# Attention and two MLPs on one core: from whole batches beside the first MLP to one half batch beside each half of it

## What is computed

```python
scores = q @ k.T / 8 + slope[h] * -|i - j|          # only 0 <= i - j < 128, the rest is masked
attn   = exp(scores - max) / (sum + 1e-9)
x      = attn @ v, heads side by side               # (4, 576, 512)
xn     = (x - mean) / sqrt(var + 1e-6) * g_ln
x      = x + relu(xn @ w_ch1) @ w_ch2               # 512 -> 2048 -> 512
h      = relu(x @ w_in)                             # 512 -> 1024
out    = (h * sigmoid(conv3(h))) @ w_out            # conv3: three taps along the positions
```

## Time and profile before

| | |
|---|---|
| median of three runs | 839.34 us |
| the profiled execution, its own time | 845.15 us |
| its span, first to last instruction | 843.4 us |
| mean granted clock of TensorE | 0.990 |
| busy: TensorE, VectorE, ScalarE, GpSimd | 812.5, 521.1, 371.9, 177.3 us |
| instructions | 17148 |
| chain that ended last | TensorE 80%, issue 9%, VectorE 7%, ScalarE 2%, GpSimd 1% |

### The profile page before, as it was taken

One profiled execution on the slowest core, in us unless ns is written; L12 is line 12 of the kernel. 1 busy time (PEld: TensorE's weight loads), 2 busy tenths in 40 slices (PEclk: granted clock), 3 DMA queues, 4 the chain that ended last, 5 costly groups with the idle time before them and its releaser, 6 DMA issues.

```text
span 843.4 us, 17148 instructions
## 1 busy us (share of the span) xinstructions
PE 812.5 (96%) x5871; PEld 770.4 (91%) x5871; DVE 521.1 (62%) x1420; ACT 371.9 (44%) x1031; POOL 177.3 (21%) x170
## 2 busy tenths in 40 slices
PE   9999877999989999998999999999999999999998
PEld 5668776999979999998999999999998999999998
DVE  2556665777447777745677764422228977788862
ACT  4626543566323556522466541222325544444442
POOL 5437772122012112101022110011110110111100
PEclk9999999999989999999999999999999999999999
DMA  5415432222031222112212301411212022221201
GB/s 145 121 45 155 129 85 85 71 74 67 3 120 38 63 72 72 37 58 67 65 50 57 100 9 57 136 57 41 88 52 85 22 79 84 77 77 35 70 23 43
DMA packets 56111, 59.30 MB, mean 70 GB/s; under 512 B 24800, under 2 KB 43232, under 8 KB 55520
## 3 DMA queue, kind: packets, MB, share of 16 engines
q1 hardware_dynamic: 56032, 58.30, 23.4%
HBM read 44.12 MB, written 14.16 MB: 69 GB/s over the span
## 4 chain that ended last, share of the span: by engine, by line
PE 80%; issue 9%; DVE 7%; ACT 2%; POOL 1%; ACTq 0%; DVEq 0%; POOLq 0%
PE bank L1303 22%; PE bank L1305 20%; PE bank L1304 20%; PE bank L1274 3%; PE bank L1242 3%; PE bank L1256 3%; PE bank L1203 2%; PE bank L1194 2%; PE bank L1227 2%; PE bank L1216 1%; PE bank L1286 1%; DVE q_st L1054 1%; PE bank L1295 1%; ACT prob L744 1%; DVE prob L966 1%
## 5 line engine op out<-in xcount | busy, mean ns | idle before, releaser
L1303 PE MATMUL bank<-xn_hi,wa_hi 128*128 128x288 f32 x512 | 158.1, 309 | 3.4 <-issue 1.9
L1303 PE MATMUL bank<-h_hi,wb_hi 128*128 128x288 f32 x512 | 158.3, 309 | 0.5 <-DVE ch_stage L1034 0.5
L1304 PE MATMUL bank<-xn_lo,wa_hi 128*128 128x288 f32 x512 | 152.7, 298 | 0.0
L1305 PE MATMUL bank<-xn_hi,wa_lo 128*128 128x288 f32 x512 | 152.4, 298 | 0.0
L1304 PE MATMUL bank<-h_lo,wb_hi 128*128 128x288 f32 x512 | 151.7, 296 | 0.0
L1305 PE MATMUL bank<-h_hi,wb_lo 128*128 128x288 f32 x512 | 151.5, 296 | 0.0
L1023 DVE SCALAR_TENSOR_TENSOR h_lo<-bank,h_hi 128x288 fp32r<-128x288 f32 x128 | 58.3, 455 | 120.2 <-ACT h_hi L774 118.8
L774 ACT ACTIVATE h_hi<-bank 128x288 fp32r<-128x288 f32 x128 | 52.5, 410 | 176.2 <-PE bank L1305 175.3
L1303 PEld LDWEIGHTS bank<-xn_hi,wa_hi 128*128 128x128 f32 x512 | 97.6, 191 | 7.3 <-issue 5.0
L1303 PEld LDWEIGHTS bank<-h_hi,wb_hi 128*128 128x128 f32 x512 | 97.2, 190 | 4.5 <-issue 2.9
L1304 PEld LDWEIGHTS bank<-xn_lo,wa_hi 128*128 128x128 f32 x512 | 97.8, 191 | 0.0
(11 more groups left out here) (127 smaller groups left out, 1721.3 us busy)
## 6 DMA issues: line engine op xcount, KB each, us to landing
w_stage<-w SPq DMA_DIRECT2D x32, 256.0 KB, 2.9
k_raw<-qkT SPq DMA_DIRECT2D x48, 144.0 KB, 2.9
q_raw<-qkT SPq DMA_DIRECT2D x48, 144.0 KB, 2.9
x_in<-x_spill SPq DMA_DIRECT2D x8, 580.0 KB, 4.4
ch_in<-ch_spill SPq DMA_DIRECT2D x8, 580.0 KB, 5.3
x_spill<-xT SPq DMA_DIRECT2D x4, 1152.0 KB, 4.2
ch_spill<-ch_stage SPq DMA_DIRECT2D x32, 144.0 KB, 2.1
out<-out_stage SPq DMA_DIRECT2D x32, 144.0 KB, 1.8
```

What stands on the lines that cost most here:

```text
L1303: nc.tensor.matmul(dst, w_h, a_h, start=start, stop=False)
L1304: nc.tensor.matmul(dst, w_h, a_l, start=False, stop=False)
L1305: last = nc.tensor.matmul(dst, w_l, a_h, start=False, stop=stop)
```

## The change

Each phase holds one chunk's MLP (16 steps, 32 slots) and one chunk's attention, always the next one:

| phase | MLP | attention |
|---|---|---|
| prologue | none | batch 0, chunk 0 (plain float32, as before) |
| first | batch 0, chunk 0 | batch 0, chunk 1 (now split) |
| loop of 3 passes: one | batch b, chunk 1 | batch b + 1, chunk 0 |
| zero | batch b + 1, chunk 0 | batch b + 1, chunk 1 |
| last | batch 3, chunk 1 | none |

Core of the diff (the functions are rewritten to take batch and chunk):

```diff
-FRAME = {("PT", "A"): 0.0, ("S", "A"): 1.0, ("PT", "B"): 1.01, ("S", "B"): 2.0, ("O", "A"): 3.0, ("S", "C"): 4.0, ("O", "B"): 5.0}
-FIRST_NORM, FIRST_HEAD, HEAD_SLOTS, LAST_NORM = 0.0, 6.5, 5.2, 55.5
-STEPS = 2 * F1
+STEPS = F1
+TILES = ([(128, 0, 128, 128, 0), (128, 0, 256, 0, 128), (64, 128, 192, 0, 384)],
+         [(128, 0, 256, 0, 0), (128, 128, 256, 0, 256)])
+GROUPS = ([[(0, 0), (1, 128)], [(2, 0)]], [[(0, 0), (1, 256)]])
+PARTS = ([(0, 128, 0, 256, 0), (1, 128, 256, 192, 128), (2, 64, 448, 64, 256)],
+         [(1, 128, 128, 256, 0), (0, 128, 0, 128, 0), (2, 128, 384, 128, 128)])
+HEAD0, HEAD_SLOT = 0.9, 2.6
+AT = {("S", 0): 0.0, ("S", 1): 1.1, ("PT", 0): 2.95, ("O", 0): 4.35}
+D_NORM = (1.8, 1.4)
+PREP_AT, PREPV_AT = 1.5, 2.0
+NORM_AT = 24.2
+NORM_TIMES = {("IN", 0): 0.0, ("IN", 1): 1.0, ("OUT", 0): 2.8, ("IN", 2): 3.3, ("OUT", 1): 4.2, ("OUT", 2): 5.2}
-WARM = [(1.79, 8)] + [(m + 0.78, 4) for m in range(2, H)] + ...
+WARM = [(1.79, 8)] + [(m + 0.78, 3) for m in range(2, H)] + ...
-W_PROLOGUE = 8
-FIRST_W, W_SLOTS, W_PACE = 0.9, 1.15, 0.85
+W_PROLOGUE = 10
+FIRST_W, W_SLOT, W_PACE = 0.9, 0.95, 1.1
...
+    if kind != "last":
+        c = ATT_C[kind]
+        out += head_items(c, HEAD0, HEAD_SLOT, AT) + norm_items(NORM_AT, NORM_TIMES)
+        out += [(HEAD0 + HEAD_SLOT * (h - 1) + PREP_AT if h else -0.95, ("PREP", h)) for h in range(H)]
+    if kind == "first":
+        out += [(0.25 + W_PACE * (n - W_PROLOGUE), ("W", n)) for n in range(W_PROLOGUE, NW1)]
...
+        def phases(run, eng):
+            run("prologue", None, 0)
+            run("first", 0, 0)
+            with eng.Fori(0, B - 1) as b:
+                run("one", b, b + 1)
+                run("zero", b + 1, b + 1)
+            run("last", B - 1, None)
...
+            def load_qk(b, c, h):
...
+                sp.dma_start(qk_raw[:, h % 2, :, 0:KEYS[c]], qkT[b, h, :, :, KEY0[c]:KEY0[c] + KEYS[c]]).then_inc(qk_loaded[h % 2], 16)
...
+                sp.dma_start(ch_dram[b, :, :, CH * c:CH * (c + 1)], ch_stage[:]).then_inc(ch_spilled, 16)
...
+            def prob_t_hi(b, c, h):
...
+                nc.scalar.activation(pt_hi[:], bank_of(b, c, ("PT", h, 0))[:], ACT.Copy).then_inc(pt_hi_ready, 1)
...
+                    delays = [("Y", 0.5, "y"), ("PREP", 0, "qk_hi"), ("PREPV", 0, "v_hi"), ("S", 0.4, "exps"), ("PT", 0.3, "pt"),
+                              ("O", 0.3, "o"), ("OUT", 0.3, "norm"), ("A", 0, "relu"), ("B", 0, "evac"), ("W", 0, "w")]
...
+                    delays = [("Y", 0, "y"), ("PREP", 0.1, "q_lo"), ("S", 0.2, "min"), ("S", D_NORM[ca or 0], "normalise"), ("PT", 0.5, "pt"),
+                              ("O", 0.4, "o"), ("IN", 0.2, "stats"), ("IN", 1.1, "apply"), ("OUT", 0.6, "norm_lo"),
+                              ("A", 0.1, "relu"), ("B", 0, "evac"), ("W", 0.3, "w")]
```

1265 lines of the change are left out of this document (528 added, 737 removed).

## The result

The changed kernel takes **892.17 us** (median of 4, 889.37 to 892.98) against 840.13 us for the kernel before on the same chip: a ratio of 1.061, 95% interval 1.058 to 1.065. I had said 849 (815 to 868). The direction was right, the loss was forecast at a fifth of its size (9.7 us of 52), and the time lies outside the range.

The account below looks back on a forecast made before the run. TensorE's own work plus its waits was taken as the bound: floor 806.8 + 19.2 + 7.2 + 12.8 + 3.5 + 3.6 = 853.1 us on the span, put at 849 on the median, slower by 1.2%; range 815 to 868.

Parts of the forecast that it names:

- The prologue: Stage before the first MLP: six fillers off -1.7, early score group off -1.0, two more weight tiles nothing; 56.8 us (56 to 60).
- (a): Chunk-0 phases: the queues' closed chain of waits takes 7.1 us a head against TensorE's 6.3; +19.2 us (0 to 31).
- (f): Transfers on SP: fewer per head and spill, queries loaded two heads ahead; no TensorE wait expected, nothing added to the sum.
- (b): Chunk-1 phases: only outputs now and then wait for pt_lo behind a relu, 0.3 us a head; +7.2 us (0 to 19).
- (c): First phase: GpSimd without slack, VectorE's normalise beside its low parts, 1.6 us a head; +12.8 us (3 to 27).
- (d): Phase ends: next phase's input stands 0.75 slot behind the last head's outputs; 7 x 0.5 = +3.5 us (0 to 10).
- (e): Loop edges: two back edges instead of one, 1.8 us each; +3.6 us against the 1.8 taken out of the floor.
- The third rival: Narrow f32r matmuls are dear: 0.13 us more on four matmuls of 32 chunk-1 heads, +17; 866 us median; chance 11%.
- The queues keep up: Rival: (a) and (b) vanish and the first phase costs 10.4; 820 us median, faster by 2.3%; chance 31%.

Follow-up runs that it names:

- r3_slot28: Changed kernel with heads 2.8 instead of 2.6 slots apart and norms 1.6 slots later; chunk-0 phases 3.5 us longer, chunk-1 phases 6.6 longer, first phase 5.5 shorter.
- r5_s1_early: Changed kernel with a chunk-0 head's second score group right behind the first (0.05 instead of 1.1 slots); three chunk-0 phases 247.2 us instead of 250.6.
- r7_s1_q_pt: Changed kernel with second scores right behind the first, queries' copy before keys' high part, transposes 0.35 and outputs 0.25 slot later; three chunk-0 phases 233.0 us instead of 250.6.
- l1_weights_first: Changed kernel with the second load of the second MLP's input behind five more weight-tile loads; last phase 50.8 us instead of 55.7, ratio interval 1.039 to 1.050.
- c3_combined: r7_s1_q_pt with chunk-0 normalisation at 1.0 slots, eight prologue weight tiles 1.15 heads apart and the edit of l1_weights_first; 850.0 us, ratio interval 1.007 to 1.013.

## Why the prediction was right or wrong

Three terms of the sum failed. The prologue's two more tiles were put at nothing, and six fillers counted as time to be had back: +10.9 us. The ring (a) was right in its mechanism and too short: 0.8 us a head over TensorE's own work, measured 1.44, +18.2 for the three phases. And (f), the transfers, stands in the sum at nothing: +4.6.

**What bounds the kernel** was read rightly: TensorE's own work, plus what it waits for. The three forecast waits (probabilities, low part of the transposes, sum of the outputs) are among those listed; the scores' wait for the low half of the queries I had only inside the ring.

**The prologue: the step failed in its sign.** I took six fillers off at 1.13 us for four and said that "ScalarE and GpSimd have room, so nothing is added" for two more tiles. The fillers are not idle time that can be had back: with three instead of four and tiles closer together the granted clock fell in nine of twelve profiles, and the prologue took 60.8 to 67.9 us: 3 to 11 us lost for the 1.7 saved. With the clock up the prologue is 56.4 to 57.8, against my 56.8. The bounds, 56 to 60, left that state out altogether, though the earlier trace rows had a lower clock in plain sight (0.97 in batch 0's run) and I had named it there.

**(a), the chunk-0 ring: right mechanism, size off.** Ring 7.74 us and not 7.1. The parts that I had summed to 6.85 are there, 0.14 longer in all (normalise 1.49 for my 1.3, the way from the first minima to pt_hi 1.33 for 1.2, the others a little shorter). What was too small is the share of the relus. I added 0.25; in the rows above one low part takes 0.37 in line (344.58 to 344.95) and one high part holds the second exp back by as much (its minima end at 348.26, it starts at 348.63), 0.75 together. Over the floor the ring makes 1.44 a head, 34.6 for 24 heads, where I had 19.2; the phases lost 250.6 - 3 x 70.5 = 39. Even my upper bound, 1.3 a head with "all relus in the ring", was too low. I also took the sum as the pace of the kernel and did not see that TensorE's own places form part of the ring; r3_slot28, r5_s1_early and r7_s1_q_pt showed that.

**(b), chunk-1 phases: right by two errors.** 73.6 us against my 73.05. But the floor under it was wrong. TensorE, a chunk-1 head of the changed kernel, groups that nothing holds up, first instruction of the group and of what follows:

```profile
264.29 0.28 PE L1013 MATMUL bank<-k_hi,q_st 128*128 128x256 f32 x1
...
264.75 0.29 PE L1071 MATMUL bank<-h_hi,wb_hi 128*128 128x288 f32 x1
...
265.55 0.60 PE L1028 MATMUL bank<-ident,prob 128*128 128x128 f32 x4
265.90 0.38 PE L1071 MATMUL bank<-xn_hi,wa_hi 128*128 128x288 f32 x1
...
293.34 0.35 PE L1047 MATMUL bank<-pt_hi,v_st 128*128 128x256 f32 x1
...
293.66 0.22 PE L1047 MATMUL bank<-pt_hi,v_st 128*128 128x128 f32 x1
...
294.05 0.35 PE L1071 MATMUL bank<-h_hi,wb_hi 128*128 128x288 f32 x1
```

0.46 + 0.35 + 0.71 = 1.52 a head. I had 1.95, from durations in the chain of waits (0.73, 0.55, 0.67), which for scores and transposes include the tail that the next group covers. So the floor of such a phase is 51.05 + 8 x 1.52 + 2.1 (six norm groups of 0.35) = 65.3 and not 69, and it lost 8.3 us and not the 4 that I forecast. The chunk-0 head was right by the same accident: 0.63 + 0.68 + 0.86 = 2.17 in the trace, where I had subtracted that 1.95 from a 4.1 that had waits of its own in it: from start to start the groups of a whole head take 3.47 us in the loop of before (scores 0.47, 0.47 and 0.18, transposes 0.35 and 0.68, outputs 0.66 twice). Over the 32 chunk-1 heads that is 14 us of floor too much, and 14 us of waiting too little. With this floor the changed kernel had more to give than I thought, and lost more.

**(c), the first phase**: +2.5 on 82.3, near by the same two errors: over its floor of 65.3 the phase lost 19.5 us, where I had 13.3. Its signs were right: VectorE beside GpSimd's low parts, and GpSimd busy over 50 us. The low half of the queries there took up to 1.39 us in r7_s1_q_pt's trace.

**(d) and (e)** aren't told apart by any run; the two loop edges of the changed kernel's profile are 1.1 and 1.4 us of TensorE's time, 2.5 where (e) had 3.6.

**(f), put at nothing, failed.** I had written that "No wait of TensorE on a transfer is among these rows" and looked at the loads of the heads. The load that hurt stands behind a wait of its own queue: the second load of the second MLP's input waits for the low part of the first, and the weight tiles stand behind it. Before, those tiles were spread over the second half of a phase of 64 slots; now they share 32 slots with those loads. 4.6 us over my number, and all of it came back in l1_weights_first.

**The rivals.** The narrow f32r matmuls are not dear: four transposes take 0.35, and the four 128-column matmuls from 293.66 to 294.05 take 0.10 each. My 0.11 was right for them, or a little high. But taking the padding off isn't free: the last two outputs of a chunk-0 head, of 64 columns and 64 rows, take 0.17 each (349.44 to 349.78), and the outputs of a whole head, 1.32 us before, are now 0.71 + 0.86 = 1.57. That is 0.25 a whole head, 0.20 of it in chunk 0, and it is in the floors above. The third rival looked for it in chunk 1. The Trainium skill, page "TensorE: Matmul & The Clock Gate", section "Back-to-back issue gap", gives about 81 ns for a stream of weight load and 128-column matmul; the trace's 88 and 98 ns lie between that and my 0.11. "The queues keep up" was refuted by the 7.74 us. The range failed because its dearest end was one rival's price alone, while all five stages ahead of the second MLP missed upwards at once.

## What to carry to other kernels

Read the floor of a group from start to start and not from its duration in a chain, and write the ring of a head down as one list with every instruction that stands in line on each engine, the other work's included, and with TensorE's own places. Filler on TensorE is not slack: before taking it off, or before adding work that can make TensorE wait, read the granted clock of several executions: one that stayed up doesn't say that the next one will. And when a schedule's phase is cut in half, follow each queue past its waits: what stands behind a wait moves with it.

## What I had not expected of the hardware

From 25 us on the same prologue code kept its granted clock at 1.00 in three profiles and fell to 0.50 in nine, with a wait of 1.8 us or more in both kinds; the kernel's times spread by 12.6 us from it and from what else varied, where c3_combined's, whose clock stays up, spread by 1.9. And a three-column operation of VectorE took 0.73 us beside a GpSimd subtraction. At the end of the last phase a 128x512 subtraction of VectorE, 0.69 us elsewhere, took 2.78 beside GpSimd's 2.70, and ended 0.55 after it:

```profile
658.98 2.70 POOL L529 TENSOR_TENSOR y_lo<-x_in,y_hi 128x1160 fp32r<-128x1160 f32 x1 [1.42 <-ACT y_hi L646]
```

```profile
659.45 2.78 DVE L846 TENSOR_TENSOR wa_lo<-w_stage,wa_hi 128x512 fp32r<-128x512 f32 x1 [1.12 <-ACT wa_hi L642]
```

What stays open: which of the two, the thinner filler or the wait, brings the clock down, since no profile with either edit fell, and how far the chip matters, since no edited prologue was profiled on chips 7 or 10, where the unedited one fell each time; and what else lies between 842 us and the floor, of which the chunk-0 and the chunk-1 phases hold some 6 us each and the first phase some 14.
